# Three weight pieces split later: their high parts behind the eighth linear step, their low parts behind block 1's convolution

## The chip, the cores and the metric

The kernel runs on one core of a Trainium2 chip. The metric is the device time of one execution in microseconds, lower is better. Five engines of the core work side by side, each on its own list of instructions, and wait for one another only through semaphores: TensorE (PE in the profile), VectorE (DVE), ScalarE (ACT), GpSimd (POOL) and SyncE (SP), which issues most of the transfers.

## What is computed

Three layers run over 8192 tokens of 192 values, all in float32: a convolution over the last 7 tokens whose weights are a softmax per token and head, a layer with a rational activation, and a gated layer behind an RMS norm.

```python
def _attn_ref(x, weight_gen):            # x (2, 4096, 192), weight_gen (2, 4096, 8, 7)
    w = np.exp(weight_gen - max over the 7 taps);  w = w / (sum + 1e-09)
    out[b, s, h, g] = sum over k of w[b, s, h, k] * x_pad[b, s + k, h, g]
def _moe_ref(x, w_in, w_out, a, b):      # 192 -> 2048 -> 192
    h = x @ w_in
    P = a[0] + a[1]*h + a[2]*h*h + a[3]*h*h*h
    Q = 1.0 + np.abs(b[0])*np.abs(h) + np.abs(b[1])*h*h
    return (P / (Q + 1e-6)) @ w_out
def _moe2_ref(x, w_gate, w_val, w_out, rms_g):   # 192 -> 1536 -> 192
    xn = x / rms(x) * rms_g
    g = xn @ w_gate
    return ((g * (1.0 / (1.0 + np.exp(-g)))) * (xn @ w_val)) @ w_out
```

## The kernel before

The tokens are cut into 16 blocks of 512. A block passes through all three layers and everything between them stays on the chip. The blocks overlap: each engine has an order written out by hand (`PE_PROGRAM`, `ACT_PROGRAM`, `DVE_PROGRAM`, `POOL_PROGRAM`), which `run_iterations` repeats. An entry is a step, its number and a lag: in iteration i the step works on block i minus lag. So the layer of block 0 with the rational activation, which has lag 1, begins in iteration 1 and ends in iteration 2 (lag 2), and the gated layer has lags 2 and 3. The first iterations and the last are written out and leave out steps whose block isn't there; the ones between are a loop.

The first layer of both feed-forward layers is five matmuls of reduced precision that together give float32: each weight matrix and the input are split into a high part (rounded to float32r) and a low part (the rest). The splitting of the weights happens once, before the loop settles. `PIECES` lists eight pieces. Pieces 0 to 3 are `w_in`; pieces 4 to 7 are `w_gate` and `w_val`, 128 x 1536 each. SyncE loads a piece into a staging place, `piece_high` (ACT, L448) copies it to the high part, and `piece_low` subtracts the high part from the staged piece: on DVE for pieces 0 to 3 (L544), on POOL for pieces 4 to 7 (L383). The first matmul that needs pieces 4 to 7 is gate 0 of block 0; it waits for four low parts on the semaphore `wlo` (`LOWS`). One more user waits on `wlo` for the first of them: root 0 of block 0, since piece 4 is staged in `seed`, which root writes.

The steps around the change, of the rational layer of a block, for chunks c of 0 to 15 and pairs q of chunks:

- up1 c (PE, L672 to L676): five matmuls into a PSUM bank. The bank is taken again only after its reader is done.
- linear c (ACT, L469 and L471): two activations of 512 columns from that bank.
- horner c (DVE, L596, L597, L599): three instructions, each with one operand in PSUM.
- abs q (ACT, L476), root t (ACT, L484, for two pairs), square q (ACT, L490).
- py q (DVE, L612), qy q (DVE, L607), newton q (DVE, L618): one instruction of 1024 columns each, both large operands in SBUF.
- down1 c (PE, L681).

In iteration 1 the order on DVE is horner 0 to 5, py 0, py 1, qy 0, horner 6, horner 7, qy 1, newton 0, newton 1, horner 8, 9, 10, py 2, qy 2, horner 11, newton 2, qy 3, and then in iteration 2 py 3, horner 12, newton 3.

On POOL the work of a block is its convolution: seven products (`mul`, L403 and L407) and additions (`add`, L416; the last one, `add 6`, is L418 and L421), all 128 x 768 with two inputs in SBUF. Block 0's convolution is done on DVE ahead of all this. Block 1's is done on POOL: mul 0 to 6 and add 1 to 5 stand in iteration 1, add 6 at the head of iteration 2. mul 0 of block 1 waits for that block's rows of x, `x_in`, which SyncE loads behind all weight pieces and behind the first `w_out` (L342), in `load_first(1)`: one transfer of 768 KB and two of 94.5 KB for the halo. After them SyncE issues `w_blk` (L345) and the second `w_out` (L347).

Before the change ACT runs piece_high 0 to 4, x_high 0 and 1, piece_high 5, and in iteration 0 piece_high 6 and 7, all ahead of linear 0 of block 0. POOL runs piece_low 4 to 7 ahead of block 1's convolution.

Of the kernel before, what the change touches and what calls it, by code (L numbers as in the profile page):

```python
# [25 lines left out]
def program(text):  # L26

    steps = [entry.split() for line in text.strip().splitlines() for entry in line.split(",") if entry.strip()]
    return [(name, int(n), int(lag)) for name, n, lag in steps]
# [12 lines left out]

ACT_PROGRAM = program("""
square 4 2, x_high 1 1, square 5 2, abs 6 2, silu 0 3, silu 1 3, abs 7 2, silu 2 3, silu 3 3, exp 0 0,
linear 0 1, root 3 2, square 6 2, silu 4 3, linear 1 1, piece 6 0, square 7 2, linear 2 1, linear 3 1,
piece 7 0, abs 0 1, linear 4 1, silu 5 3, linear 5 1, abs 1 1, root 0 1, square 0 1, square 1 1, linear 6 1,
silu 6 3, abs 2 1, linear 7 1, ss 0 2, silu 7 3, abs 3 1, silu 8 3, root 1 1, linear 8 1, linear 9 1,
linear 10 1, square 2 1, silu 9 3, abs 4 1, silu 10 3, linear 11 1, silu 11 3, square 3 1, xn_high 0 2,
abs 5 1, xn_high 1 2, linear 12 1, linear 13 1, root 2 1, linear 14 1, x_high 0 0, linear 15 1, y 0 3,
""")  # L50
# [8 lines left out]
""")  # L59

POOL_PROGRAM = program("""
add 6 1, less 0 0, norm 0 0, mul 0 0, mul 1 0, mul 2 0, add 1 0, mul 3 0, add 2 0, mul 4 0, rms 0 2, add 3 0,
mul 5 0, add 4 0, mul 6 0, add 5 0,
""")

# [34 lines left out]
def run_iterations(eng, order, ops, last):  # L100

    trail = max(lag for _, _, lag in order)

    def iteration(i):
        for name, n, lag in order:
            if name in ONCE:
                there = isinstance(i, int) and i == lag
            elif isinstance(i, int):
                there = FROM_BLOCK.get(name, 0) <= i - lag <= last
            else:  # L110
                there = True
            if there:
                ops[name](i - lag, n)

    for i in range(trail + 1):
        iteration(i)
    with eng.Fori(trail + 1, last) as i:
        iteration(i)
    for i in range(last, last + trail + 1):
        iteration(i)  # L120


def wait(eng, sem, value):

    if not isinstance(value, int) or value > 0:
        eng.wait_ge(sem, value)


def build(nc, x, weight_gen, w_in, w_out, a, b, w_gate, w_val, w2_out, rms_g, out):
# [7 lines left out]
    LAST = NBLK - 1  # L137
# [9 lines left out]
    with ctx:  # L147
        def sb(name, shape, dt=F32):
            return ctx.enter_context(nc.sbuf_tensor(name, shape, dt))
# [27 lines left out]
        square = sb("square", [P, SLOTS, D])  # L177
# [4 lines left out]
        rms = sb("rms", [P, 4, SLOTS])  # L182
# [81 lines left out]
        BY_DVE = 4  # L264
# [6 lines left out]
        def taps_of(k, blk):  # L271

            early = isinstance(blk, int) and blk < 2
            return (w_first[:, blk * SLOTS * HK:(blk + 1) * SLOTS * HK] if early else w_blk[:, :]).rearrange("p (a k) -> p a k", k=K)[:, :, k:k + 1]\
                .broadcast_to([P, SLOTS * H, D // H])

        def rows_of(k):
            return x_in[:, k * D:k * D + ROW].rearrange("p (a g) -> p a g", g=D // H)

        def by_head(rows):  # L280
            return rows.rearrange("p (a g) -> p a g", g=D // H)
# [5 lines left out]
        def slots(rows):  # L287
            return rows.rearrange("p (j d) -> p j d", j=SLOTS)

        def slot_heads(rows):  # L290
            return rows.rearrange("p (j h) g -> p j h g", h=H)

        def x_count(blk):
            return blk * 16 + 80 if not isinstance(blk, int) or blk else 48
# [6 lines left out]
        def soft_count(blk):  # L301
            return blk if not isinstance(blk, int) or blk else 1
# [4 lines left out]
        def less_peak(eng, blk):  # L307
            taps, peak, _ = soft(blk)
            wait(eng, sm_peak, soft_count(blk))
            eng.tensor_tensor(taps, taps, over_taps(peak, taps), ALU.subtract).then_inc(sm_less, 1)  # L310

        def normalise(eng, blk):
            taps, _, total = soft(blk)
            wait(eng, sm_inverse, soft_count(blk))
            eng.tensor_tensor(taps, taps, over_taps(total, taps), ALU.mult).then_inc(sm_norm, 1)
# [56 lines left out]
        @block.gpsimd  # L372
        def _(pool):
            pool.memset(x_in[:, 0:HALO * D], 0.0).then_inc(halo0, 1)
            pool.memset(ident[:, :], 0.0).then_inc(consts, 1)
            pool.memset(MINUS_HALF, -0.5).then_inc(consts, 1)
            pool.wait_ge(consts, 2)
            pool.affine_select(out=ident[:, :], in_=ident[:, :], compare_op=ALU.not_equal, fill=1.0,
                               base=0, pattern=[[-1, P]], channel_multiplier=1).then_inc(consts, 1)

            def piece_low(_, n):
                pool.wait_ge(whi, n + 1)
                pool.tensor_tensor(PIECES[n][3], PIECES[n][1], PIECES[n][2], ALU.subtract).then_inc(wlo, 1)  # L383

            def peak_taken_off(blk, _):
                less_peak(pool, blk)

            def normalised_taps(blk, _):
                normalise(pool, blk)

            pool.wait_ge(conv0_ready, 1)
            pool.memset(x_in[:, 0:(HALO - SLOTS) * D], 0.0).then_inc(halo0, 1)
            pool.wait_ge(wlo0, BY_DVE)
            for n in range(BY_DVE, len(PIECES)):
                piece_low(0, n)


            def tap_product(blk, k):
                if k == 0:
                    wait(pool, x_in_ready, x_count(blk))  # L400
                    wait(pool, sm_norm, soft_count(blk))
                    wait(pool, xt_ready, blk * 2)
                    pool.tensor_tensor(conv_heads, slot_heads(rows_of(0)), slot_heads(taps_of(0, blk)), ALU.mult)                        .then_inc(tap_ready, 1)  # L403
                else:
                    if k >= 3:
                        wait(pool, tap_sum, (blk - 1) * (K - 2) + k - 2)
                    pool.tensor_tensor(by_head(prod[:, k % 2, :]), rows_of(k), taps_of(k, blk), ALU.mult)\  # L407
                        .then_inc(tap_ready, 1)

            def tap_add(blk, k):  # L410
                wait(pool, tap_ready, (blk - 1) * K + k + 1)
                if k > 1:
                    wait(pool, tap_sum, (blk - 1) * (K - 2) + k - 1)
                product = slots(prod[:, k % 2, :])
                if k < K - 1:
                    pool.tensor_tensor(conv_rows, conv_rows, product, ALU.add).then_inc(tap_sum, 1)  # L416
                else:
                    pool.tensor_tensor(conv_twice, conv[:, :, DA:D], product[:, :, DA:D], ALU.add)\  # L418
                        .then_inc(twice_ready, 1)
                    wait(pool, twice_ready, blk)  # L420
                    pool.tensor_tensor(conv_rows, conv_rows, product, ALU.add).then_inc(conv_ready, 1)  # L421

            def rms_inverse(blk, _):
                wait(pool, ss_ready, blk + 1)
                pool.sem_inc(pool_turn, 1)
                pool.tensor_scalar(MEAN_SQ, SUM_SQ, 1.0 / D, EPS_RMS, ALU.mult, ALU.add).then_inc(mean_ready, 1)
                wait(pool, mean_ready, blk + 1)
                pool.tensor_tensor(RMS_INV, MEAN_SQ, MINUS_HALF, ALU.pow).then_inc(rms_ready, 1)

            run_iterations(pool, POOL_PROGRAM, {"mul": tap_product, "add": tap_add, "rms": rms_inverse,  # L430
                                                "less": peak_taken_off, "norm": normalised_taps}, LAST)

        @block.scalar
        def _(act):
# [8 lines left out]
            def exponentials(blk, _):  # L443
                taps, _, _ = soft(blk)
                wait(act, sm_less, soft_count(blk))
                act.activation(taps, taps, ACT.Exp).then_inc(sm_exp, 1)

            def piece_high(_, n):  # L448
                act.wait_ge(piece_in[n], 16 * len(PIECES[n][0]))
                act.activation(PIECES[n][2], PIECES[n][1], ACT.Copy).then_inc(whi, 1)  # L450

            def x_high(blk, part):
                wait(act, h_ready, blk * 16)
                wait(act, xt_ready, blk * 2 + (part + 1))
                act.activation((x_ah, x_b)[part][:, :], bank[XPOSE_BANK[part]][:, :], ACT.Copy).then_inc(xt_hi, 1)
# [3 lines left out]
                piece_high(0, n)  # L459
            x_high(0, 0)  # L460
            x_high(0, 1)
            piece_high(0, 5)
            act.wait_ge(coefs, 2)

            def linear(blk, c):
# [317 lines left out]
```

## Time and profile before

| | us |
|---|---|
| median of 3 runs | 1444.98 |
| lowest, highest | 1443.11, 1447.46 |
| the profiled execution, its own time | 1445.34 |
| span in its trace | 1443.5 |
| PE busy | 1368.5 (95%) |
| DVE busy | 1247.1 (86%) |
| ACT busy | 1071.0 (74%) |
| POOL busy | 458.4 (32%) |

The span runs from the first to the last instruction in the trace; the execution's own time is 1.84 us longer, and it lies 0.36 us above the median. Busy shares are means over a start, a long steady part and an end, so the rows are read by stretches. Times in the rows are microseconds from the start of the span.

### The profile page before, as it was taken

To read this page: it belongs to the slowest core of one execution; us is meant where nothing else is said; L and a number is where in the kernel's file an instruction comes from. 1 tells how busy PE (TensorE), PEld (TensorE's weight loads), DVE (VectorE), ACT (ScalarE), POOL (GpSimd) and SP (SyncE) were. 2 spreads that over 40 slices of the span, in tenths; PEclk is the share of its full clock that TensorE was granted. 3 is DMA by queue.
4 is the path that set the end of the run, shared out by engine and by line. 5 is a ranking of instruction groups with operands and counts; after the bars stand their busy time and mean duration, and the time that the engine had idled before them with its cause. 6 is when DMAs were issued, how large, how long until landed. Compare 5 with 4: busy or idle time off the path is not lost.

```text
span 1443.5 us, 20421 instructions
## 1 busy us (share of the span) xinstructions
PE 1368.5 (95%) x7040; PEld 1221.0 (85%) x7040; DVE 1247.1 (86%) x1524; ACT 1071.0 (74%) x1387; POOL 458.4 (32%) x283
## 2 busy tenths in 40 slices
PE   2676999999999999999999999999999999999999
PEld 2465898888898888889898888989888898998988
DVE  6999998989889898988989899898989989888621
ACT  4676877878787787888778788877878787777521
POOL 2935240434324143432414343241434314200000
PEclk9788999999999999999999999999999999999999
DMA  8200001000000100000010000001000000000000
GB/s 232 82 0 31 1 2 41 1 32 11 30 11 0 41 0 30 11 30 11 0 41 0 30 11 30 11 0 41 0 30 11 30 12 0 12 0 1 12 12 11
DMA packets 12514, 32.30 MB, mean 22 GB/s; under 512 B 1604, under 2 KB 7234, under 8 KB 12480
## 3 DMA queue, kind: packets, MB, share of 16 engines
q1 hardware_dynamic: 11744, 31.61, 6.8%
q8 instruction: 21, 0.34, 0.1%
q10 hardware_dynamic: 736, 0.23, 0.1%
q14 instruction: 13, 0.11, 0.0%
HBM read 25.55 MB, written 6.29 MB: 22 GB/s over the span
## 4 chain that ended last, share of the span: by engine, by line
PE 76%; DVE 11%; ACT 7%; issue 4%; DMA 2%; SPq 0%; ACTq 0%; POOL 0%; DVEq 0%; POOLq 0%
PE dn L681 32%; PE bank L672 9%; PE bank L673 8%; PE bank L674 8%; PE bank L675 8%; PE bank L676 8%; DVE den L607 4%; ACT seed L484 2%; PE bank L688 2%; DVE num L599 2%; DVE num L596 1%; DVE num L612 1%; DVE num L618 1%; ACT L484 1%; DMA glu<-in_moe_w_val_dram 1%
## 5 line engine op out<-in xcount | busy, mean ns | idle before, releaser
L681 PE MATMUL dn<-dn_w,num 128*128 128x192 f32 x2048 | 378.8, 329 | 17.1 <-DVE num L618 9.9
L681 PEld LDWEIGHTS dn<-dn_w,num 128*128 128x128 f32 x2048 | 343.5, 192 | 24.3 <-DVE num L618 8.6
L469 ACT ACTIVATE den<-bank,coef 128x512 f32<-128x512 f32 x256 | 175.5, 686 | 175.8 <-PE bank L676 164.6
L681 PE MATMUL dn<-dn_w,glu 128*128 128x192 f32 x1536 | 280.8, 327 | 5.3 <-DVE glu L643 5.3
L681 PEld LDWEIGHTS dn<-dn_w,glu 128*128 128x128 f32 x1536 | 254.3, 190 | 12.9 <-DVE glu L643 8.9
L596 DVE TENSOR_TENSOR num<-num,bank 128x512 f32<-128x512 f32 x256 | 173.9, 679 | 70.1 <-ACT num L471 68.1
L612 DVE SCALAR_TENSOR_TENSOR num<-num,coef,seed 128x1024 f32<-128x1024 f32 x128 | 183.5, 1435 | 40.8 <-ACT seed L490 40.3
L471 ACT ACTIVATE num<-bank,coef 128x512 f32<-128x512 f32 x256 | 199.5, 779 | 0.0
L618 DVE SCALAR_TENSOR_TENSOR num<-den,num 128x1024 f32<-128x1024 f32 x128 | 193.1, 1510 | 0.0
L597 DVE SCALAR_TENSOR_TENSOR den<-den,coef,bank 128x512 f32<-128x512 f32 x256 | 188.9, 738 | 0.0
L599 DVE SCALAR_TENSOR_TENSOR num<-num,coef,bank 128x512 f32<-128x512 f32 x256 | 188.9, 738 | 0.0
L643 DVE TENSOR_TENSOR glu<-glu,bank 128x512 f32<-128x512 f32 x192 | 130.5, 680 | 66.1 <-PE bank L676 64.9
L607 DVE SCALAR_TENSOR_TENSOR den<-den,seed 128x1024 f32<-128x1024 f32 x128 | 181.5, 1419 | 0.0
L510 ACT ACTIVATE glu<-bank 128x512 f32<-128x512 f32 x192 | 113.0, 597 | 81.5 <-PE bank L676 76.5
L416 POOL TENSOR_TENSOR conv<-conv,prod 128x768 f32<-128x768 f32 x75 | 170.2, 2270 | 0.0
L672 PE MATMUL bank<-xn_ah,up_ah 128*128 128x512 f32 x384 | 162.7, 424 | 0.0
L476 ACT ACTIVATE den<-den 128x1024 f32<-128x1024 f32 x128 | 134.9, 1054 | 30.3 <-DVE num L599 30.3
L407 POOL TENSOR_TENSOR prod<-x_in,w_blk 128x768 f32<-128x768 f32 x84 | 154.5, 1847 | 4.4
L673 PE MATMUL bank<-xn_al,up_ah 128*128 128x512 f32 x384 | 150.1, 391 | 0.0
L674 PE MATMUL bank<-xn_ah,up_al 128*128 128x512 f32 x384 | 150.0, 391 | 0.0
L675 PE MATMUL bank<-xn_b,up_bh 128*128 128x512 f32 x384 | 149.7, 390 | 0.0
L676 PE MATMUL bank<-xn_b,up_bl 128*128 128x512 f32 x384 | 149.6, 389 | 0.0
(86 smaller groups left out, 1983.4 us busy)
## 6 DMA issues: line engine op xcount, KB each, us to landing
x_in<-in_x_dram SPq DMA_DIRECT2D x14, 960.0 KB
out_dram<-y_out SPq DMA_DIRECT2D x16, 384.0 KB, 2.3
w_blk<-in_weight_gen_dram SPq DMA_DIRECT2D x14, 112.0 KB, 2.0
dn_w<-in_moe_w_out_dram SPq DMA_DIRECT2D x1, 1536.0 KB, 20.7
dn_w<-in_moe_w_out_dram SPq DMA_DIRECT2D x1, 1152.0 KB, 10.6
num<-in_moe_w_in_dram SPq DMA_DIRECT2D x1, 768.0 KB, 6.6
num<-in_moe_w_in_dram SPq DMA_DIRECT2D x2, 384.0 KB, 8.2
seed<-in_moe_w_gate_dram SPq DMA_DIRECT2D x1, 768.0 KB, 10.0
```

The costliest lines, as they stand in the source:

```text
L471: act.activation(chunk(num, c), h, ACT.Identity, scale=na(3), bias=na(2)).then_inc(lin_ready, 1)
L597: dve.scalar_tensor_tensor(d, d, B_ABS[:, 0:1], h, ALU.add, ALU.mult)
L599: dve.scalar_tensor_tensor(n, n, na(1), h, ALU.add, ALU.mult).then_inc(poly_ready, 1)
L607: dve.scalar_tensor_tensor(d, d, EPS_Q, y, ALU.add, ALU.mult).then_inc(qy_ready, 1)
L612: dve.scalar_tensor_tensor(n, n, na(0), y, ALU.add, ALU.mult).then_inc(py_ready, 1)
L618: dve.scalar_tensor_tensor(n, d, -2.0, n, ALU.add, ALU.mult).then_inc(act_ready, 1)
L672: pe.matmul(out_bank[:, :], ah, m_ah[:, :], start=True, stop=False)
L673: pe.matmul(out_bank[:, :], ah, m_al[:, :], start=False, stop=False)
L674: pe.matmul(out_bank[:, :], al, m_ah[:, :], start=False, stop=False)
L675: pe.matmul(out_bank[:, :], bh, m_b[:, :], start=False, stop=False)
L676: return pe.matmul(out_bank[:, :], bl, m_b[:, :], start=False, stop=True)
L681: done = pe.matmul(banks[:, j // 2, j % 2 * D:(j % 2 + 1) * D], acts[:, j * P:(j + 1) * P], w, start=first and j % 2 == 0, stop=last, skip ...
```

## The change

The high parts of pieces 5, 6 and 7 leave their places ahead of linear 0. In ACT's order they stand in iteration 1: piece 5 behind linear 7, piece 6 behind abs 3, piece 7 behind root 1. The low parts of pieces 5, 6 and 7 leave their place ahead of block 1's convolution on POOL and stand at the head of iteration 2, behind add 6 of block 1 and ahead of `less`. Piece 4 stays where it was. No instruction is added or removed, and SyncE's list is the same.

```diff
--- before.py
+++ after.py
@@ -42,9 +42,9 @@
 
 ACT_PROGRAM = program("""
 square 4 2, x_high 1 1, square 5 2, abs 6 2, silu 0 3, silu 1 3, abs 7 2, silu 2 3, silu 3 3, exp 0 0,
-linear 0 1, root 3 2, square 6 2, silu 4 3, linear 1 1, piece 6 0, square 7 2, linear 2 1, linear 3 1,
-piece 7 0, abs 0 1, linear 4 1, silu 5 3, linear 5 1, abs 1 1, root 0 1, square 0 1, square 1 1, linear 6 1,
-silu 6 3, abs 2 1, linear 7 1, ss 0 2, silu 7 3, abs 3 1, silu 8 3, root 1 1, linear 8 1, linear 9 1,
+linear 0 1, root 3 2, square 6 2, silu 4 3, linear 1 1, square 7 2, linear 2 1, linear 3 1,
+abs 0 1, linear 4 1, silu 5 3, linear 5 1, abs 1 1, root 0 1, square 0 1, square 1 1, linear 6 1,
+silu 6 3, abs 2 1, linear 7 1, piece 5 1, ss 0 2, silu 7 3, abs 3 1, piece 6 1, silu 8 3, root 1 1, piece 7 1, linear 8 1, linear 9 1,
 linear 10 1, square 2 1, silu 9 3, abs 4 1, silu 10 3, linear 11 1, silu 11 3, square 3 1, xn_high 0 2,
 abs 5 1, xn_high 1 2, linear 12 1, linear 13 1, root 2 1, linear 14 1, x_high 0 0, linear 15 1, y 0 3,
 """)
@@ -59,7 +59,7 @@
 """)
 
 POOL_PROGRAM = program("""
-add 6 1, less 0 0, norm 0 0, mul 0 0, mul 1 0, mul 2 0, add 1 0, mul 3 0, add 2 0, mul 4 0, rms 0 2, add 3 0,
+add 6 1, piece 5 2, piece 6 2, piece 7 2, less 0 0, norm 0 0, mul 0 0, mul 1 0, mul 2 0, add 1 0, mul 3 0, add 2 0, mul 4 0, rms 0 2, add 3 0,
 mul 5 0, add 4 0, mul 6 0, add 5 0,
 """)
 
@@ -391,8 +391,7 @@
             pool.wait_ge(conv0_ready, 1)
             pool.memset(x_in[:, 0:(HALO - SLOTS) * D], 0.0).then_inc(halo0, 1)
             pool.wait_ge(wlo0, BY_DVE)
-            for n in range(BY_DVE, len(PIECES)):
-                piece_low(0, n)
+            piece_low(0, BY_DVE)
 
 
             def tap_product(blk, k):
@@ -428,7 +427,8 @@
                 pool.tensor_tensor(RMS_INV, MEAN_SQ, MINUS_HALF, ALU.pow).then_inc(rms_ready, 1)
 
             run_iterations(pool, POOL_PROGRAM, {"mul": tap_product, "add": tap_add, "rms": rms_inverse,
-                                                "less": peak_taken_off, "norm": normalised_taps}, LAST)
+                                                "less": peak_taken_off, "norm": normalised_taps,
+                                                "piece": piece_low}, LAST)
 
         @block.scalar
         def _(act):
@@ -459,7 +459,6 @@
                 piece_high(0, n)
             x_high(0, 0)
             x_high(0, 1)
-            piece_high(0, 5)
             act.wait_ge(coefs, 2)
 
             def linear(blk, c):
```

## Rows read from the trace of the kernel before

**Rows 1.** The page: busy time, share of the span and instructions of each engine.

```profile
PE 1368.5 (95%) x7040; PEld 1221.0 (85%) x7040; DVE 1247.1 (86%) x1524; ACT 1071.0 (74%) x1387; POOL 458.4 (32%) x283
```

**Rows 2.** Windows: stretch, its length, busy us (instructions) by engine, clock, DMA share, GB/s.

```profile
120.00:150.00 30.00, 19.66 (x91) 16.41 (x90) 30.00 (x32) 20.95 (x34) 14.92 (x9) 0.89 0.11 37
300.00:400.00 100.00, 99.55 (x525) 89.26 (x524) 89.55 (x112) 76.29 (x100) 33.42 (x21) 1.00 0.08 26
```

**Rows 3.** Timeline of PE: start, duration, instruction, and the idle time before it.

```profile
27.76 0.63 PE L676 MATMUL bank<-x_b,up_bl 128*128 128x512 f32 x1
33.08 0.40 PE L676 MATMUL bank<-x_b,up_bl 128*128 128x512 f32 x1
...
150.99 0.59 PE L672 MATMUL bank<-x_ah,up_ah 128*128 128x512 f32 x1 [2.30 <-DVE xn_al L634]
```

**Rows 4.** Timeline of ACT, 31 to 64 us.

```profile
31.91 1.49 ACT L450 ACTIVATE up_bh<-glu 128x1536 fp32r<-128x1536 f32 x1 [1.92 <-DMA glu<-in_moe_w_val_dram]
33.30 0.67 ACT L469 ACTIVATE den<-bank,coef 128x512 f32<-128x512 f32 x1
...
41.77 0.77 ACT L471 ACTIVATE num<-bank,coef 128x512 f32<-128x512 f32 x1
...
59.57 1.06 ACT L476 ACTIVATE den<-den 128x1024 f32<-128x1024 f32 x1 [7.27 <-DVE num L599]
61.68 2.00 ACT L484 ACTIVATE seed<-den,coef 128x2048 f32<-128x2048 f32 x1 [1.05 <-DVE den L607]
```

**Rows 5.** Timeline of DVE: the first horner steps of block 0.

```profile
34.67 0.69 DVE L596 TENSOR_TENSOR num<-num,bank 128x512 f32<-128x512 f32 x1 [5.40 <-ACT num L471]
...
36.59 0.68 DVE L596 TENSOR_TENSOR num<-num,bank 128x512 f32<-128x512 f32 x1
```

**Rows 6.** Timeline of DVE: py, qy and newton while POOL convolves (first is two instructions).

```profile
47.95 5.03 DVE L612 SCALAR_TENSOR_TENSOR num<-num,coef,seed 128x1024 f32<-128x1024 f32 x2 [1.70 <-ACT seed L490]
52.89 2.82 DVE L607 SCALAR_TENSOR_TENSOR den<-den,seed 128x1024 f32<-128x1024 f32 x1
```

**Rows 7.** Timeline of POOL over the same time.

```profile
47.57 1.83 POOL L416 TENSOR_TENSOR conv<-conv,prod 128x768 f32<-128x768 f32 x1
49.48 2.41 POOL L407 TENSOR_TENSOR prod<-x_in,w_first 128x768 f32<-128x768 f32 x1
51.85 2.78 POOL L416 TENSOR_TENSOR conv<-conv,prod 128x768 f32<-128x768 f32 x1
```

**Rows 8.** Timeline of POOL: piece 4's low part, first product and last addition of block 1.

```profile
29.36 3.47 POOL L383 TENSOR_TENSOR up_al<-seed,up_ah 128x1536 fp32r<-128x1536 f32 x1 [6.51 <-DVE up_bl L544]
...
39.65 3.45 POOL L383 TENSOR_TENSOR up_bl<-glu,up_bh 128x1536 fp32r<-128x1536 f32 x1
43.06 1.54 POOL L403 TENSOR_TENSOR conv<-x_in,w_first 128x768 f32<-128x768 f32 x1
44.57 3.03 POOL L407 TENSOR_TENSOR prod<-x_in,w_first 128x768 f32<-128x768 f32 x2
...
69.48 1.83 POOL L421 TENSOR_TENSOR conv<-conv,prod 128x768 f32<-128x768 f32 x1
```

**Rows 9.** Timeline of DVE: py 2, py 3 and the start of horner 12.

```profile
72.50 1.27 DVE L612 SCALAR_TENSOR_TENSOR num<-num,coef,seed 128x1024 f32<-128x1024 f32 x1
...
79.02 1.27 DVE L612 SCALAR_TENSOR_TENSOR num<-num,coef,seed 128x1024 f32<-128x1024 f32 x1
80.22 0.67 DVE L596 TENSOR_TENSOR num<-num,bank 128x512 f32<-128x512 f32 x1
```

**Rows 10.** DMA packets by size, from 37 to 38 us, then from 38 to 39 us.

```profile
DMA packets 240, 0.30 MB, mean 303 GB/s; under 512 B 24, under 2 KB 226, under 8 KB 240
...
DMA packets 285, 0.25 MB, mean 249 GB/s; under 512 B 15, under 2 KB 285, under 8 KB 285
```

**Rows 11.** Timeline of SyncE's issues, then w_blk's median us from issue to landing.

```profile
32.34 0.35 SPq L345 DMA_DIRECT2D w_blk<-in_weight_gen_dram  x1
...
w_blk<-in_weight_gen_dram SPq DMA_DIRECT2D x1, 112.0 KB, 7.7
```

## The prediction

> **What bounds the kernel now.** I read the page's busy line first: PE is busy for 95% of the span, DVE for 86% [rows 1]. A mean over stages doesn't say who sets the start, so the windows by stage come next. From 300 to 400 us PE is busy 99.55 of 100 us at full clock: the steady part is bound by TensorE [rows 2]. From 120 to 150 us it is the other way round: DVE is busy 30.00 of 30 us, PE 19.66 [rows 2]. Then the timeline of PE: its last idle gap of the start ends at 150.99, and DVE's `xn_al` ended it [rows 3]. So the kernel is a start that lasts to 151 us and hangs on DVE, and behind it a steady part that begins when the start is over and has its own length. A microsecond won or lost on DVE's chain in the start moves the end by one. The change touches only the start.
>
> The timelines of the start show three things.
>
> - ACT puts the high parts of pieces 5, 6, 7 ahead of linear 0. The last runs at 31.91 for 1.49 us behind a wait for its load, and linear 0 begins at 33.30 [rows 4]. Its input was there much earlier: up1 0's last matmul ran from 27.76 to 28.39 [rows 3]. DVE waited 5.40 us for that and began horner 0 at 34.67 [rows 5].
> - POOL runs four low parts of 3.45 to 3.47 us from 29.36 on, then block 1's convolution from 43.06 to 71.31, without a wait between them [rows 8].
> - While POOL convolves, DVE's py, qy and newton take twice as long or more: two py take 5.03 us and qy 0 2.82 us [rows 6]; py 2, behind the convolution, takes 1.27 us [rows 9]. POOL's operations stretch too: the product at 49.48 takes 2.41 us against 1.54 us alone, the addition at 51.85 2.78 us against 1.83 us [rows 7, 8]. The times fit taking turns. py 0 is ready at 47.95, the addition before it ends at 49.40, the next product gets its turn 2.41 - 1.54 = 0.87 us after its start, at 50.35. So each side waits until the other's instruction is over: DVE for 1.5 to 1.8 us, POOL for about 0.95 us. Horner, with one operand in PSUM, shows nothing of the kind: it took 1.92 us beside the low parts, 34.67 to 36.59 [rows 5].
>
> **Part 1: the high parts move on ACT, a gain at the front.** Linear 0 can start when up1 0 is done, 28.39 + 0.03 = 28.4 instead of 33.30. DVE's own low parts of pieces 2 and 3 are out of the way by then, so horner 0 starts 1.37 us behind linear 0 as now, at 29.8 instead of 34.67: 4.9 us earlier. Not all of it reaches py 0. PE delivers up1 3 only at 33.48 [rows 3], so linear 3 runs from 33.5 to 34.8, then abs 0 (1.06 us), linear 4 and linear 5 (1.3 us each) end at 38.4. Before, linear 5 ended at 42.54 [rows 4] and py 0 started 5.41 us later [rows 6]. The same chain of abs 1, table load, root and square gives py 0 ready at 43.8, 4.15 us earlier.
>
> The three copies, 3 x 1.49 = 4.5 us, go into ACT's gaps. Piece 5 falls into the 7.27 us before abs 3 and is free [rows 4]. Piece 6 lies in the 1.05 us before root 1, where ACT waits for qy 1 [rows 4]: in the new schedule below it ends at 56.8 and qy 1 at 56.7, so 0.1 us. Piece 7 ends at 60.3, linear 8 at 61.6, and DVE is busy until 61.95: free. If that cover failed, the most it could cost is 1.49 us for each. Nothing stands behind a new wait: the three loads had landed by 31.91 [rows 4], and `wlo` of piece 4, for which root 0 waits, comes at 32.83 as now [rows 8].
>
> **Part 2: block 1's convolution starts earlier on POOL, but not by three low parts.** POOL is free at 29.36 + 3.47 = 32.83. mul 0 waits for block 1's rows of x, though. Their 768 KB transfer is the only one then with more than 2 KB in a row (768 KB over 128 partitions is 6 KB), and 14 packets above 2 KB are still seen from 37 to 38 us; from 38 to 39 there is none [rows 10]. The halo transfers follow, and behind these `w_blk`, issued at 32.34, landed 7.7 us later, at 40.0 [rows 11]. I take 39.5 for x. The bounds are 38.0 (end of the large packets) and 43.06, where mul 0 ran without a wait [rows 8]. So the convolution gains 43.06 - 39.5 = 3.6 us, not 10.2.
>
> **Part 3: three low parts now lie beside py, qy and newton.** Before, they ran beside horner steps, at no cost. Now they start behind the convolution and fall on py 2, qy 2, newton 2, qy 3, py 3. I lay out the turns: product 1.5, addition 1.83, low part 3.45, a turn of DVE 0.95 to 1.15, horner 1.92.
>
> - mul 0 to 2 run from 39.5 to 44.0. py 0 44.0 to 45.15, add 1 to 46.8, py 1, mul 3 to 49.3, qy 0 to 50.4. Horner 6 and 7 to 54.25 beside add 2, mul 4, add 3 (to 55.55). qy 1 to 56.7, mul 5 to 58.0, newton 0, add 4 to 60.8, newton 1 to 61.95. Six turns of DVE stand in the convolution, as before, so it keeps its length of 28.25 us [rows 8] and ends at about 67.9.
> - Horner 8, 9, 10 to 67.7; py 2 was at 72.50 before [rows 9], so DVE is 4.8 us ahead here. py 2 waits for the last addition: to 69.1. Low 5 from 68.9 to 72.35, qy 2 to 73.5, horner 11 to 75.4. Low 6 from 73.3 to 76.75, newton 2 to 77.9. Low 7 from 77.7 to 81.15, qy 3 to 82.3, py 3 to 83.5.
> - Before, py 3 ended and horner 12 began at 80.22 [rows 9]. The change is 83.5 - 80.3 = +3.2 us there. A shorter count gives the same: end of x's transfer + 28.25 + 3 x 3.45 + 3 x 0.95 + 2.3 for qy 3 and py 3 = 83.25, +3.0 us. I take +3.1.
>
> This count holds no term of part 1: from py 0 on DVE takes turns with POOL, and the end hangs on when POOL is through. Behind 83.5 all steps wait for one another as before, POOL is done, and DVE's chain leads to 151 us [rows 2, 3]; gate 0, which needs all four low parts, runs far behind them.
>
> No row of before has a low part beside an instruction with two large SBUF inputs. The price of its turn lies between nothing (sum -4.6) and its whole 3.45 us (sum +3.1). The nearest row is the 128 x 768 addition, the same operation on half the columns, and DVE waited for the whole of it; I take the upper end.
>
> The Trainium skill ("SBUF — State Buffer", section "Who interferes with whom") states that a VectorE instruction with two SBUF inputs contends with a GpSimd instruction that reads SBUF, and that whichever comes first holds the shared ports for the whole instruction. It speaks against this change: by it the sum is +3.1 us; if the low parts were exempt it would be -4.6 us. The trace agrees for the convolution's operations, 2.82 us for a qy beside them; that it holds for the low parts no row shows.
>
> **The sum.** The profiled execution took 1445.34 us with a span of 1443.5. Adding 3.1 gives a span of 1446.6 and 1448.4 for such an execution. It lay 0.36 us above the median, 1444.98, so the predicted median is 1448.1, +0.21%. About 0.3%, 4.3 us, is what a measurement of this kernel can tell from no change.
>
> **The rivals.**
>
> - *Slower, the convolution starts late.* Each microsecond by which x lands later than 39.5 moves the end by one. Above 40.8 the loss passes 4.3 us; at 43.06 it is +6.6, 1451.6. For it: the large packets end shortly before 38, and no row times the landing of the halo. Against: `w_blk`, issued later, was there at 40.0 [rows 11]. The same size would come from each low part taking a turn more than it needs.
> - *Faster, the low parts don't block DVE.* Then py 2 to py 3 takes the 7.7 us of before, from 67.95 to 75.7, and the gain of the front stays: -4.6, 1440.4. For it: no row shows the contention. Against: both have two inputs in SBUF like the additions.
> - *Nearly nothing.* x lands at 38.0 (+1.5), or some of the loss is taken up before 151 us, since from py 3 on PE, ACT and POOL are ahead of DVE: -1 to +1.5, 1444 to 1446.5. Against: DVE has no idle time from 120 to 150 us [rows 2].
>
> **How the numbers follow.** Forecast, +1.5 to +4.3: 0.54. Late start: 0.22. No blocking: 0.12. Nearly nothing: 0.12. Slower by over 0.3% is the late start and a little of the forecast's upper edge, 0.26; faster is the second rival and a little noise, 0.14; the rest, 0.60, lies within 0.3%. The range leaves out the no-blocking case and the far end of the late start: 1441.8 to 1451.8.
>
> **What would show it.** Right: horner 0 near 29.8, mul 0 of block 1 near 39.5 behind an idle POOL, three low parts from 68 to 81 us with qy 2, newton 2 and qy 3 at 2.4 to 4.5 us each, and the end of PE's start near 154. Wrong: those three at 1.2 us, mul 0 before 38 or after 41, or linear 8 or root 1 late behind a copy of a piece. The prediction falls as a whole if the shift at py 3 isn't that at gate 0.

## The result and the profile after

| | before | changed |
|---|---|---|
| median of 20 runs, us | 1444.40 | 1448.47 |
| lowest, highest | 1443.04, 1447.46 | 1446.16, 1452.34 |
| span of the profiled execution | 1443.5 | 1445.1 |

The ratio is 1.0026, with a 95% interval of 1.0020 to 1.0033: the changed kernel is 3.8 us slower by this ratio, and the medians lie 4.1 us apart. The prediction was 1448.1 for the median, +0.21%. The profiled execution, 1446.86 us, lies in the lower part of the changed kernel's spread: 10 of 20 runs lie from 1446.16 to 1448.27, the others from 1448.66 to 1452.34. A second trace, below, is of an execution in the upper part. One execution among the runs below, of 3619 us (the kernel without late low parts), is left out of its ratio; its cause isn't known.

Lines of the changed kernel are one lower than before from L402 on (L611 is py, L606 qy, L617 newton, L595 the first instruction of horner). Its busy line, against [rows 1]:

```profile
PE 1367.5 (95%) x7040; PEld 1220.2 (84%) x7040; DVE 1255.6 (87%) x1524; ACT 1070.9 (74%) x1387; POOL 461.7 (32%) x283
```

The windows from 120 to 150 and 300 to 400 us, with the columns of [rows 2]:

```profile
120.00:150.00 30.00, 21.12 (x94) 18.39 (x93) 30.00 (x34) 21.07 (x31) 14.94 (x9) 0.81 0.11 37
300.00:400.00 100.00, 99.55 (x524) 89.27 (x523) 89.51 (x112) 77.38 (x101) 34.80 (x22) 1.00 0.08 26
```

DVE is busy 8.5 us longer with the same instructions; the window of the steady part is the same. The place where the start ends, in the timeline of PE, comes 2.34 us later than in [rows 3]:

```profile
153.33 0.50 PE L671 MATMUL bank<-x_ah,up_ah 128*128 128x512 f32 x1 [1.45 <-DVE xn_al L633]
```

The timeline of DVE, the steps of [rows 5, 6, 9]:

```profile
29.61 0.69 DVE L595 TENSOR_TENSOR num<-num,bank 128x512 f32<-128x512 f32 x1 [0.61 <-ACT num L470]
...
42.88 4.44 DVE L611 SCALAR_TENSOR_TENSOR num<-num,coef,seed 128x1024 f32<-128x1024 f32 x2 [1.70 <-ACT seed L489]
...
66.88 1.39 DVE L611 SCALAR_TENSOR_TENSOR num<-num,coef,seed 128x1024 f32<-128x1024 f32 x1
68.20 4.43 DVE L606 SCALAR_TENSOR_TENSOR den<-den,seed 128x1024 f32<-128x1024 f32 x1
...
74.47 2.56 DVE L617 SCALAR_TENSOR_TENSOR num<-den,num 128x1024 f32<-128x1024 f32 x1
76.95 4.48 DVE L606 SCALAR_TENSOR_TENSOR den<-den,seed 128x1024 f32<-128x1024 f32 x1
81.36 1.27 DVE L611 SCALAR_TENSOR_TENSOR num<-num,coef,seed 128x1024 f32<-128x1024 f32 x1
82.55 0.67 DVE L595 TENSOR_TENSOR num<-num,bank 128x512 f32<-128x512 f32 x1
```

And the timeline of POOL, the steps of [rows 8]:

```profile
38.95 1.54 POOL L402 TENSOR_TENSOR conv<-x_in,w_first 128x768 f32<-128x768 f32 x1 [6.35 <-DMA x_in<-in_x_dram]
...
65.36 1.84 POOL L420 TENSOR_TENSOR conv<-conv,prod 128x768 f32<-128x768 f32 x1
67.15 4.41 POOL L383 TENSOR_TENSOR up_al<-stage,up_ah 128x1536 fp32r<-128x1536 f32 x1
71.52 4.43 POOL L383 TENSOR_TENSOR up_bl<-stage,up_bh 128x1536 fp32r<-128x1536 f32 x1
75.91 4.45 POOL L383 TENSOR_TENSOR up_bl<-glu,up_bh 128x1536 fp32r<-128x1536 f32 x1
```

In the kernel before, the same three steps on DVE (qy 2, newton 2, qy 3) have nothing beside them on POOL:

```profile
73.70 1.21 DVE L607 SCALAR_TENSOR_TENSOR den<-den,seed 128x1024 f32<-128x1024 f32 x1
...
76.75 1.21 DVE L618 SCALAR_TENSOR_TENSOR num<-den,num 128x1024 f32<-128x1024 f32 x1
77.89 1.21 DVE L607 SCALAR_TENSOR_TENSOR den<-den,seed 128x1024 f32<-128x1024 f32 x1
```

At py 2 DVE is 72.50 - 66.88 = 5.6 us ahead of before [rows 9]. Then qy 2 takes 4.43 us instead of 1.21, newton 2 2.56, qy 3 4.48, each beside a low part that itself takes 4.4 us instead of 3.45 [rows 8]. At horner 12, DVE is 82.55 - 80.22 = 2.3 us behind [rows 9]. All of the loss arises in these 16 us, and the same 2.3 us are there at 153.33. (The low parts' starts lie 4.37 and 4.39 us apart, so their length doesn't hang on how the profile takes an end.)

The copies of the high parts on ACT, with root 1 between them (timeline of ACT), lie in its gaps as laid out:

```profile
47.12 1.49 ACT L450 ACTIVATE up_ah<-stage 128x1536 fp32r<-128x1536 f32 x1
...
54.63 1.47 ACT L450 ACTIVATE up_bh<-stage 128x1536 fp32r<-128x1536 f32 x1
56.05 2.00 ACT L483 ACTIVATE seed<-den,coef 128x2048 f32<-128x2048 f32 x1
57.96 1.47 ACT L450 ACTIVATE up_bh<-glu 128x1536 fp32r<-128x1536 f32 x1
```

### The profile page after: what moved, and what is told of

Its sections match the earlier page's. It is cut to its first block, busy times and chain, and to the rows that moved or that the text cites. A ratio compares the mean times of both kernels' runs of the same rounds, so it can differ in the third digit from the quotient of the medians.

```text
span 1445.1 us, 20421 instructions
## 1 busy us (share of the span) xinstructions
PE 1367.5 (95%) x7040; PEld 1220.2 (84%) x7040; DVE 1255.6 (87%) x1524; ACT 1070.9 (74%) x1387; POOL 461.7 (32%) x283
## 4 chain that ended last, share of the span: by engine, by line
PE 76%; DVE 13%; ACT 7%; issue 4%; DMA 0%; ACTq 0%; POOL 0%; DVEq 0%; SPq 0%; POOLq 0%
PE dn L680 32%; PE bank L671 9%; PE bank L672 8%; PE bank L673 8%; PE bank L674 8%; PE bank L675 8%; DVE den L606 4%; ACT seed L483 2%; PE bank L687 2%; DVE num L598 2%; DVE num L595 2%; DVE num L617 1%; DVE num L611 1%; ACT L483 1%; ACT seed L489 1%
## 5 line engine op out<-in xcount | busy, mean ns | idle before, releaser
L595 DVE TENSOR_TENSOR num<-num,bank 128x512 f32<-128x512 f32 x256 | 174.0, 680 | 65.2 <-ACT num L470 63.5
L611 DVE SCALAR_TENSOR_TENSOR num<-num,coef,seed 128x1024 f32<-128x1024 f32 x128 | 184.3, 1441 | 39.0 <-ACT seed L489 38.5
L617 DVE SCALAR_TENSOR_TENSOR num<-den,num 128x1024 f32<-128x1024 f32 x128 | 194.5, 1521 | 0.0
L606 DVE SCALAR_TENSOR_TENSOR den<-den,seed 128x1024 f32<-128x1024 f32 x128 | 188.1, 1470 | 0.0
```

Of the source, the lines that this page charges most:

```text
L595: dve.tensor_tensor(n, n, h, ALU.mult).then_inc(num1_ready, 1)
L606: dve.scalar_tensor_tensor(d, d, EPS_Q, y, ALU.add, ALU.mult).then_inc(qy_ready, 1)
L611: dve.scalar_tensor_tensor(n, n, na(0), y, ALU.add, ALU.mult).then_inc(py_ready, 1)
L617: dve.scalar_tensor_tensor(n, d, -2.0, n, ALU.add, ALU.mult).then_inc(act_ready, 1)
```

## The experiments

The theory: in the start, VectorE's instructions with two large SBUF operands take turns with GpSimd's, and the three late low parts are three turns of 3.45 us. The rivals: ScalarE's new order is at fault; or the landing of x decides alone. All runs and the two kernels stand in one table. "mul 0" is the start of block 1's convolution on POOL, "horner 12" shows the end of py 3 on DVE, "gated" is PE's first matmul behind its last gap of the start; these and the span come from one trace each, the ratio to the kernel before from the timed runs.

| kernel | ratio, 95% interval | mul 0 | horner 12 | gated | span |
|---|---|---|---|---|---|
| before | | 43.06 | 80.22 | 150.99 | 1443.5 |
| changed | 1.0026, 1.0020 to 1.0033 | 38.95 | 82.55 | 153.33 | 1445.1 |
| changed, second trace | 1.0021, 1.0012 to 1.0031 | 42.40 | 85.80 | 156.55 | 1448.3 |
| no late low parts | 0.9973, 0.9963 to 0.9983 | 38.77 | 75.93 | 146.71 | 1439.3 |
| GpSimd's half alone | 1.0030, 1.0016 to 1.0045 | 38.50 | 84.18 | 154.91 | 1446.4 |
| x first | 1.0006, 0.9997 to 1.0016 | 34.69 | 80.35 | 151.13 | 1442.7 |
| x last | 1.0046, 1.0030 to 1.0063 | 41.55 | 84.95 | 155.70 | 1448.2 |
| the three low parts behind newton 3 | 0.9995, 0.9986 to 1.0005 | 39.41 | 75.18 | 149.16 | 1441.8 |
| piece 5 put back | 1.0002, 0.9992 to 1.0012 | 38.46 | 80.89 | 151.66 | 1443.3 |
| piece 5 put back, low parts 6, 7 behind newton 3 ("the faster kernel") | 0.9974, 0.9965 to 0.9984 | 38.45 | 75.59 | 146.33 | 1439.1 |
| the faster kernel, ScalarE's order of before | 0.9996, 0.9987 to 1.0006 | 41.06 | 80.17 | 150.94 | 1442.5 |
| the faster kernel, x first | 0.9967, 0.9955 to 0.9978 | 37.09 | 76.14 | 146.90 | 1438.5 |

From "gated" to the end of the span it is 1291.5 to 1292.8 us in all of them: what the start wins or loses reaches the end. The rest goes with TensorE's granted clock just behind "gated". Its mean from there to 180 us is 0.93 to 0.95 in five traces (before, no late low parts, x last, low parts behind newton 3, the faster kernel), and these have 1292.5 to 1292.8; it is 1.00 in the other seven, and these have 1291.5 to 1291.8.

### Without the late low parts

This kernel leaves out the low parts of pieces 5, 6 and 7: zeros stand in their place, written by GpSimd ahead of everything. They count on `wlo` too, so root 0 of block 0 waits for all four counts and not for one.

```diff
+            for n in range(BY_DVE + 1, len(PIECES)):
+                pool.memset(PIECES[n][3].bitcast(F32), 0.0).then_inc(wlo, 1)
...
             def piece_low(_, n):
+                if n > BY_DVE:
+                    return
...
-                    act.wait_ge(wlo, 1)
+                    act.wait_ge(wlo, LOWS)
```

> The changed kernel with the low parts of pieces 5, 6 and 7 left out: these low parts are zero, written ahead of everything while GpSimd is idle; ScalarE's order is that of the change. If the loss comes from the turns that VectorE waits while these three low parts run (my theory), py 3 ends where py 2 of the changed kernel (66.88) plus the 7.7 us of the kernel before leads, 74.6, that is 5.6 us ahead of the kernel before, and the time is about 5 us below before, ratio 0.9965. If the loss comes from ScalarE's order (copies of pieces late for root 1 or linear 8), the time stays 2 to 4 us above before, ratio 1.0015 to 1.003. If the front doesn't count at all, the ratio is 1.000.

Measured: 0.9973. The gated matmul comes at 146.71, 6.6 us ahead of the changed kernel and 4.3 us ahead of before. DVE's timeline has qy 2 and qy 3 back at 1.21 and 1.22 us:

```profile
68.22 1.28 DVE L616 SCALAR_TENSOR_TENSOR num<-num,coef,seed 128x1024 f32<-128x1024 f32 x1
69.41 1.21 DVE L611 SCALAR_TENSOR_TENSOR den<-den,seed 128x1024 f32<-128x1024 f32 x1
...
73.60 1.22 DVE L611 SCALAR_TENSOR_TENSOR den<-den,seed 128x1024 f32<-128x1024 f32 x1
```

So the low parts are the loss, and ScalarE's order isn't: this kernel has it too. The gain is 1.3 us smaller than expected, since py 2 came at 68.22, not 66.88. In this trace the turns fell less well ahead of it: py 0 and 1 together took 5.26 us from 43.41 on, against 4.44 from 42.88 in the changed kernel.

### GpSimd's half of the change alone

Against the kernel before (`run_iterations` also gets its entry for `piece`):

```diff
-add 6 1, less 0 0, ...
+add 6 1, piece 5 2, piece 6 2, piece 7 2, less 0 0, ...
...
-            for n in range(BY_DVE, len(PIECES)):
-                piece_low(0, n)
+            piece_low(0, BY_DVE)
```

> The GpSimd half of the change alone: the three low parts behind block 1's convolution, ScalarE's order as in the kernel before. If VectorE is tied to GpSimd's turns, block 1's convolution starts near 39 and py 0 near 47.95; three products and three additions then have no turn of VectorE in them. Laid out by turns, the three low parts run from 67 to 78, two of them before py 2 is there, and py 3 ends 4.5 us behind the kernel before, ratio 1.003. If the term of part 1 (4.15 us at the front) were simply added, it would be 1.6 + 4.2 = 5.8 us and more above before in a profile, ratio 1.004 to 1.006.

Measured: 1.0030, the expected size, from five executions. py 0 started at 46.64, 3.8 us later than in the changed kernel, but the gated matmul came only 1.6 us later. The timeline of POOL, then that of DVE:

```profile
66.53 3.48 POOL L383 TENSOR_TENSOR up_al<-stage,up_ah 128x1536 fp32r<-128x1536 f32 x1
69.95 3.47 POOL L383 TENSOR_TENSOR up_bl<-stage,up_bh 128x1536 fp32r<-128x1536 f32 x1
73.39 4.41 POOL L383 TENSOR_TENSOR up_bl<-glu,up_bh 128x1536 fp32r<-128x1536 f32 x1
```

```profile
70.55 3.97 DVE L612 SCALAR_TENSOR_TENSOR num<-num,coef,seed 128x1024 f32<-128x1024 f32 x1
74.44 4.43 DVE L607 SCALAR_TENSOR_TENSOR den<-den,seed 128x1024 f32<-128x1024 f32 x1
```

One low part runs beside horner steps before py 2 is there, and only two cost a turn. (Piece 7's copy began at 30.60 here and at 31.91 before [rows 4]: the weights' landing varies too, and py 0 was 1.3 us earlier than the 47.95 of before for that.) The first part's head start of 3.8 us is worth 1.6 us here: a DVE that is earlier meets one low part more. It also shows a limit of the prediction's short count: POOL is through at 77.8, 2.6 us earlier than in the changed kernel, and yet the end is later, since more of DVE's work then lies behind it (horner 11, newton 2, qy 3 and py 3).

### x earlier and x later

First, `load_first(1)` ahead of the first `w_out`:

```diff
-            src, dst = DOWN[0]
-            sp.dma_start(dst[:, :, :], src).then_inc(down_in[0], 16)
             sp.wait_ge(conv0_ready, 1)
             load_first(1)
+            src, dst = DOWN[0]
+            sp.dma_start(dst[:, :, :], src).then_inc(down_in[0], 16)
```

> The changed kernel with the transfers of block 1's x issued ahead of the first w_out instead of behind it. x then lands behind the weight pieces only, near 34.5 instead of 38.95, and the convolution starts there. By my theory the end hangs on when GpSimd is through, one microsecond for each at first and less where turns of VectorE fall free: py 3 ends 1.5 us before to 0.0 us behind the kernel before, that is 2.3 to 3.9 us ahead of the changed kernel, ratio to before 0.999 to 1.000. If the start of the convolution doesn't matter, it is the changed kernel's 1.0026.

Measured: 1.0006, a little above the expected range, and in the trace 2.2 us ahead of the changed kernel, where 2.3 to 3.9 was expected. POOL's convolution starts 4.26 us earlier and its last low part ends at 73.96 instead of 80.36, but DVE gains only 2.2 us. Its horner steps and its other work behind the last low part take what they take, however early POOL is through.

```profile
34.69 1.54 POOL L402 TENSOR_TENSOR conv<-x_in,w_first 128x768 f32<-128x768 f32 x1 [1.77 <-DMA x_in<-in_x_dram]
...
69.57 4.39 POOL L383 TENSOR_TENSOR up_bl<-glu,up_bh 128x1536 fp32r<-128x1536 f32 x1
```

Then the second `w_out` ahead of it:

```diff
+            src, dst = DOWN[1]
+            sp.dma_start(dst[:, :, :], src).then_inc(down_in[1], 16)
             sp.wait_ge(conv0_ready, 1)
             load_first(1)
...
-            src, dst = DOWN[1]
-            sp.dma_start(dst[:, :, :], src).then_inc(down_in[1], 16)
```

> The changed kernel with the transfer of the second w_out (1152 KB) issued ahead of block 1's x instead of behind it. x lands 3 to 4 us later, at 42 to 43. Laid out by turns, a convolution that starts at 42 to 42.5 ends py 3 5.0 to 5.5 us behind the kernel before (one that starts at 43 falls otherwise among the turns and gives 2.7): ratio 1.004, with 1.002 as the lower edge. If the landing of x doesn't matter, 1.0026, as it is in the changed kernel. A late x is also what could lie behind the changed kernel's slower half of executions, near 1450.

Measured: 1.0046, from four executions. mul 0 starts at 41.55, 2.6 us later than in the changed kernel, and the gated matmul comes 2.4 us later. Now qy 3 and py 3 both wait for a low part (py 3 in DVE's timeline):

```profile
80.60 4.43 DVE L611 SCALAR_TENSOR_TENSOR num<-num,coef,seed 128x1024 f32<-128x1024 f32 x1
```

### The changed kernel once more

> The changed kernel itself once more, for the spread of its executions (1446.2 to 1452.3, half of them near 1446.5 and half near 1450, where the kernel before has 1443.0 to 1447.5) and for a second trace. By my theory a trace near 1450 shows block 1's x landing later or the turns falling otherwise between 43 and 81 us, with the first matmul of the gated layer 3 us later than 153.3; a rival is TensorE's clock, which would leave that matmul in its place and cost the time behind it.

Its second trace is from an execution of 1450.08 us. Its timelines of SyncE, of POOL and of PE, in this order: the issue of x, the wait for it, and the end of the start.

```profile
22.09 11.46 SPq L331 DMA_DIRECT2D x_in<-in_x_dram  x1
```

```profile
42.40 1.54 POOL L402 TENSOR_TENSOR conv<-x_in,w_first 128x768 f32<-128x768 f32 x1 [8.59 <-DMA x_in<-in_x_dram]
```

```profile
156.55 0.50 PE L671 MATMUL bank<-x_ah,up_ah 128*128 128x512 f32 x1 [1.53 <-DVE xn_al L633]
```

The same issue took 8.63 us in the first trace:

```profile
22.12 8.63 SPq L331 DMA_DIRECT2D x_in<-in_x_dram  x1
```

x lands 3.4 us later with the same list of transfers, the gated matmul comes 3.2 us later, and the span is 3.2 us longer. It is the picture of the kernel with x last: qy 3 and py 3 both wait for a low part. x isn't all that is late here: piece 4's low part starts at 30.32 instead of 29.09 and py 0 at 44.49 instead of 42.88, so this trace alone doesn't tell a late x from late weights. The kernel with x last does: its py 0 is at 43.15, and it loses nearly as much. TensorE's clock doesn't explain it: from the gated matmul to the end it is 1291.8 us in both traces. How often this happens is less certain: of the ten executions of this run only the one traced lies above 1448.3 us (1450.08), where it was 10 of 20 in the first comparison. In the kernel before, x that lands at 42.4 is still in time for a convolution that starts at 43.06 [rows 8].

### Other places for the late low parts

The three low parts wait for newton 3:

```diff
                 pool.wait_ge(whi, n + 1)
+                if n == 5:
+                    pool.wait_ge(act_ready, 4)
```

> The changed kernel with the three low parts waiting for newton 3 of block 0. Behind it VectorE runs horner 13 to 15, a reduction and both x_low, 7.5 us with no instruction of two large SBUF operands. Two low parts (6.9 us) lie beside them, the third in py 4 and qy 4 of the next stretch, and the softmax step behind it on GpSimd is 3 us late. By my theory the gain is that of the kernel without low parts, 5 us, less 1 to 3.5 us: ratio 0.9965 to 0.999. If ScalarE's order is at fault, the ratio stays at 1.0015 to 1.003. If low parts slow VectorE whatever it runs, the ratio stays near 1.0026.

Measured: 0.9995, just above what was expected (0.9965 to 0.999), with an interval of 0.9986 to 1.0005. py 3 is as early as without low parts (horner 12 at 75.18), two low parts are free, and the third meets py 4 (timeline of POOL, then of DVE):

```profile
85.30 3.45 POOL L385 TENSOR_TENSOR up_bl<-glu,up_bh 128x1536 fp32r<-128x1536 f32 x1
```

```profile
85.70 4.12 DVE L613 SCALAR_TENSOR_TENSOR num<-num,coef,seed 128x1024 f32<-128x1024 f32 x1
```

py 4 takes 2.8 us more than its 1.28 without a low part beside it, and the gated matmul is 2.8 us later than in the faster kernel below.

Piece 5 put back, high and low:

```diff
-... linear 7 1, piece 5 1, ss 0 2, ...
+... linear 7 1, ss 0 2, ...
...
-add 6 1, piece 5 2, piece 6 2, piece 7 2, ...
+add 6 1, piece 6 2, piece 7 2, ...
...
             piece_low(0, BY_DVE)
+            piece_low(0, BY_DVE + 1)
...
             x_high(0, 1)
+            piece_high(0, 5)
```

> The changed kernel with piece 5 put back: its high part behind x_high 1 on ScalarE, its low part behind piece 4's on GpSimd, where it runs from 32.8 to 36.2 in the 6.35 us in which GpSimd waits for block 1's x. Pieces 6 and 7 stay where the change has them. By my theory one turn of 3.45 us less behind the convolution: py 3 ends 1.1 us behind to 0.6 us ahead of the kernel before, against 2.3 behind in the changed kernel; ratio 0.9995 to 1.001. If the number of late low parts isn't the cause, 1.0026.

Measured: 1.0002. Low part 5 fits into POOL's wait for x, which shrinks from 6.35 to 2.43 us, and mul 0 is no later:

```profile
32.50 3.53 POOL L383 TENSOR_TENSOR up_al<-stage,up_ah 128x1536 fp32r<-128x1536 f32 x1
38.46 1.54 POOL L403 TENSOR_TENSOR conv<-x_in,w_first 128x768 f32<-128x768 f32 x1 [2.43 <-DMA x_in<-in_x_dram]
```

Both together (piece 5 put back, the wait at n == 6):

> As the one with piece 5 put back, and the low parts of pieces 6 and 7 wait for newton 3 of block 0, so that both (6.9 us) lie beside horner 13 to 15, the reduction and x_low (7.5 us). By my theory no low part costs VectorE a turn, and the first matmul of the gated layer comes where the kernel without late low parts has it, 146.7 us (150.99 before, 153.33 changed): a span near 1439.5, ratio 0.997, faster than both. If a low part slows VectorE also beside horner steps, ratio 0.999 to 1.001.

Measured: 0.9974, 1440.40 us, faster than both kernels. The two low parts lie beside horner 13 to 15, the reduction and x_low, and neither side is any longer for it (POOL, then DVE):

```profile
78.86 3.47 POOL L385 TENSOR_TENSOR up_bl<-stage,up_bh 128x1536 fp32r<-128x1536 f32 x1 [12.18 <-DVE num L621]
82.28 3.46 POOL L385 TENSOR_TENSOR up_bl<-glu,up_bh 128x1536 fp32r<-128x1536 f32 x1
```

```profile
81.15 0.74 DVE L600 SCALAR_TENSOR_TENSOR den<-den,coef,bank 128x512 f32<-128x512 f32 x1
...
86.11 1.28 DVE L615 SCALAR_TENSOR_TENSOR num<-num,coef,seed 128x1024 f32<-128x1024 f32 x1
```

The interval overlaps that of the kernel without late low parts (0.9973), so in these places they cost nothing that can be measured.

### What the front is worth by itself

That faster kernel with `ACT_PROGRAM` of the kernel before (`piece 6 0` behind linear 1 and `piece 7 0` behind linear 3, which run in iteration 0, ahead of linear 0 of block 0):

> The faster kernel (piece 5 put back, low parts 6 and 7 behind newton 3) with ScalarE's order of the kernel before: all high parts ahead of linear 0. It says what part 1 of the change, the front on ScalarE, is worth when no late low part stands in the way. py 0 would be ready near 47, the convolution starts at 38.5 to 39. By turns py 3 ends 1.5 to 1.9 us ahead of the kernel before, against 4.6 for the same kernel with the front: first matmul of the gated layer near 149.3 and a ratio of 0.999, so the front is worth about 3 us. If the front counts for nothing here either, the ratio is 0.997; if it counts in full (4.3 us), 1.000.

Measured: 0.9996, against 0.9974 with the front. The difference is 3.2 us of 1444.4; in the traces it is 150.94 - 146.33 = 4.6 us, of which 0.9 us is a later load of piece 7 (horner 0 at 35.57, 34.67 before [rows 5]). So the front is worth 3.2 us by the times and 3.7 by the traces, not far from its full 4.15, where the low parts are out of the way. In this trace mul 0 was late too, at 41.06.

And the faster kernel with x first, the edit as above:

> The faster kernel with block 1's x issued ahead of the first w_out: the convolution starts at 36 behind piece 5's low part instead of 38.45. In the changed kernel an earlier x was worth 2 us, since the late low parts end as much earlier. With no late low part in VectorE's way, the turns in the convolution number the same whenever it starts, and by my theory it is worth 0.0 to 0.6 us here: ratio 0.9965 to 0.997. If an early x is worth something for itself, 2 us or more below the faster kernel: 0.9955 or less.

Measured: 0.9967, whose interval overlaps that of the same kernel with x behind `w_out` (0.9974). mul 0 starts 1.4 us earlier in the trace, and the gated matmul is not earlier (146.90 and 146.33). So without late low parts no gain from an earlier x is shown; the times put it at 1.0 us, within their noise.

## Why the prediction was right, point by point

- **The start hangs on DVE, the rest on PE.** Right. "gated" moved by 2.3 us with horner 12, and from there to the end all kernels take 1291.5 to 1292.8 us. The span moved only by 1.6, since the steady part was 0.7 us shorter in this trace (1291.8 us against 1292.5): in the window from 150 to 180 us TensorE's granted clock was 0.94 before and 1.00 in the changed kernel, and the twelve traces above split by the same sign.
- **Part 1, the front.** Horner 0 was forecast at 29.8 and came at 29.61. py 0 was forecast at 43.8 and came at 42.88, since the prediction took up1 3's end from before: the matmuls got shorter earlier here, from 0.63 to 0.40 us at 29.16 and in before at 31.93, and linear 3 began at 32.31 and not at 33.5. The granted clock in the changed kernel's windows is 1.00 on both sides of that step (26 to 28.5 and 29.5 to 33 us), so what shortens them isn't shown. Piece 6 was to end with qy 1: root 1 starts at 56.05, as soon as both are over. Piece 7 cost nothing: its copy is over at 59.43, linear 8 at 60.68, and DVE takes up horner 8 at 61.14, as soon as newton 1 is done.
- **Part 2, x.** Forecast at 39.5, 38.95 in this trace. The step that was mis-sized is its spread. I gave a late x 0.22 as a rival; the second trace has 42.40, and 10 of the changed kernel's 20 runs (1 of 10 in the later run) lie above 1448.3. That each microsecond by which x lands later moves the end by one held for a late x (3.45 us later, gated 3.2 later; x last 2.6 and 2.4) and only by half for an early one (4.26 and 2.2).
- **The number.** That 1448.1 lies 0.4 us from the median is in part luck. For an execution like the profiled one the prediction had 1448.4 us and a span of 1446.6; with x near its forecast place it took 1446.86 and 1445.1. The 1.5 us are 0.8 at "gated" (+2.3 where +3.1 was forecast) and 0.7 behind it. Executions near 1450 us bring the median up again. The measured change of the median is 4.1 us. The 0.3% given as what a measurement can tell from no change was too coarse as well: the interval of 1.0020 to 1.0033 tells 0.26% from none.
- **Part 3, the turns.** The convolution was to end at 67.9, and ended at 67.2. The order of turns was as laid out: py 2 just behind the last addition, low 5, qy 2, horner 11 beside low 6, newton 2, low 7, qy 3, py 3. End of py 3: 83.5 forecast, 82.6 measured; horner 12 against before +3.2 and +2.3. The upper end for a low part's price was right: qy 3 takes 4.48 us, 3.27 us above its 1.21 alone. The Trainium skill ("SBUF — State Buffer", section "Who interferes with whom") says that the one who comes second waits for the whole instruction; the trace agrees. The Trainium skill says in the same section that a VectorE instruction with at most one SBUF input, outside the 2-port modes, doesn't contend; that agrees as well, with 0.74 us for horner beside a low part in the faster kernel and 0.73 with POOL idle.
- **"This count holds no term of part 1."** Too strong. GpSimd's half alone ends 1.6 us later in the trace than the whole change, and without late low parts the front counts nearly in full. The short count (end of x + 43.75) holds only near the schedule it was made for: x first starts 4.26 us earlier and gains 2.2.
- **The rivals.** "Faster, the low parts don't block" fell by the first experiment: without them the gain of the front appears, 1440.69 us, where 1440.4 was given for it. "Slower, x late" is what the second trace shows, at 1450.08 us; 10 of the first 20 executions lie above 1448.3 us, but none of these 10 has a trace, so their cause is argued from that one and from the kernel with x last. "Nearly nothing", by slack ahead of 151 us, has no support: the 2.3 us are there undiminished.

## What to carry to other kernels

Before work is moved to a second engine that takes turns with the bounding one, as GpSimd does with VectorE here, list what the bounding engine runs in that stretch: low parts beside VectorE instructions with one SBUF operand were free, beside those with two a low part cost up to 3.3 of its 3.45 us. A wait taken off the front is worth something only if the work moved for it finds a free place too; here the same edit went from +0.26% to -0.26% when one piece stayed and two got other places. A start that waits for a load inherits that load's spread, so look at the load's landing in more than one execution.

## What the runs showed of the hardware

- With both engines waiting, the turns alternate one instruction at a time: behind a low part on POOL, DVE got one instruction, and POOL's next waited about 1 us for it (4.41 to 4.45 us instead of 3.45). In no trace did two low parts run one after the other while DVE had a two-operand instruction ready.
- The issue of one 768 KB transfer on SyncE's queue, behind the weight pieces and the first `w_out`, took 7.88 to 11.46 us in the nine traces with the same list of transfers. In the eight of them where mul 0 waits for x, it starts at 38.45 to 39.41 behind an issue of 7.88 to 8.99 us (six traces), at 41.06 behind one of 10.16 and at 42.40 behind one of 11.46. It isn't this transfer that takes the time: in each list the issue right behind the first `w_out` does. With x first, x's issue took 0.33 us and that of `w_blk`, 112 KB, 10.19 and 12.65; with x last, the second `w_out` took 13.94. What decides the spread stays open; no run was made for it.
